# One engine makes the low halves of g: a two-layer MLP behind a dynamic convolution

## The reference

```python
w = softmax(weight_gen, axis=-1)            # (4, 4096, 8 heads, 7 taps)
x_pad = 6 zero rows + x                     # causal, x is (4, 4096, 192)
conv[s, head, :] = sum_k w[s, head, k] * x_pad[s + k, head, :]   # 24 columns per head
h = conv @ w_in                             # 192 -> 2048
g = max(0.01 * h, h)
out = g @ w_out                             # 2048 -> 192, float32
```

## Time and profile before

| | |
|---|---|
| median of 3 runs | 1031.0 us (1030.97 to 1031.47) |
| profiled execution, its own time | 1031.87 us |
| its span, first to last instruction | 1030.1 us |
| granted TensorE clock over the span | 1.000 of full speed |
| busy: TensorE, VectorE, ScalarE, GpSimd | 1020.6, 939.0, 634.3, 550.5 us |

### The profile page before, as it was taken

The page is one execution under the profiler, slowest core; times in us unless marked ns, Lnnn a source line. Parts: engine busy times, 40 slices in busy tenths (PEclk is TensorE's granted clock), DMA queues, the critical chain, the costliest instruction groups (busy, mean ns, idle before and its releaser), DMA issues.

```text
span 1030.1 us, 28954 instructions
## 1 busy us (share of the span) xinstructions
PE 1020.6 (99%) x12745; PEld 612.6 (59%) x12745; DVE 939.0 (91%) x1199; ACT 634.3 (62%) x1352; POOL 550.5 (53%) x375
## 2 busy tenths in 40 slices
PE   8999999999999999999999999999999999999998
PEld 3666655556556556655655655655565565566566
DVE  8989999999999999999999999999999999998611
ACT  7966665665556656556656555665565665566564
POOL 0114665555556655655655665565665566556543
PEclk9999999999999999999999999999999999999999
DMA  9421303112021310212112121210313112111100
GB/s 266 111 62 32 98 19 98 35 40 89 4 97 35 97 35 23 77 34 98 35 38 77 20 97 35 85 45 4 98 35 97 35 31 69 34 35 36 34 17 17
DMA packets 68309, 59.84 MB, mean 58 GB/s; under 512 B 56348, under 2 KB 60700, under 8 KB 66200
## 3 DMA queue, kind: packets, MB, share of 16 engines
q1 hardware_dynamic: 67196, 55.35, 18.4%
q0 software_dynamic: 864, 2.36, 1.3%
q10 hardware_dynamic: 124, 0.29, 0.1%
HBM read 29.34 MB, written 12.58 MB: 41 GB/s over the span
## 4 chain that ended last, share of the span: by engine, by line
PE 90%; DVE 6%; DMA 1%; ACT 1%; SPq 1%; issue 0%; POOL 0%; DVEq 0%; POOLq 0%
PE h_ps L1066 43%; PE out_ps L1176 22%; PE t_ps L1176 22%; PE out_ps L1130 1%; DVE prod L681 1%; PE h_ps L1048 1%; DMA rawO<-in_moe_w_out_dram 1%; DVE gl L883 1%; DVE conv L697 1%; PE out_ps L1140 1%; DMA prod<-prod 0%; DVE gl L755 0%; ACT g L483 0%; SPq L380 0%; ACT gh L481 0%
## 5 line engine op out<-in xcount | busy, mean ns | idle before, releaser
L349 POOL TENSOR_TENSOR gl<-g,gh 128x512 f16<-128x512 f32 x360 | 543.2, 1535 | 411.4 <-ACT g L483 411.4
L481 ACT ACTIVATE gh<-h_ps 128x512 f16<-128x512 f32 x512 | 317.6, 620 | 370.2 <-PE h_ps L1066 361.0
L1176 PE MATMUL t_ps<-wo,gh 64*128 64x384 f16 (+1 forms) x1984 | 386.6, 317 | 0.9 <-ACT gh L481 0.9
L1176 PE MATMUL out_ps<-wo,gh 64*128 64x384 f16 (+1 forms) x1984 | 386.6, 317 | 0.0
L1066 PE MATMUL h_ps<-xT,whA 64*128 64x512 f16 x1920 | 364.3, 376 | 0.0
L483 ACT ACTIVATE g<-h_ps 128x512 f32<-128x512 f32 x512 | 321.9, 629 | 0.0
L681 DVE TENSOR_TENSOR prod<-xbuf,taps 128x768 f32<-128x768 f32 x186 | 273.3, 1485 | 0.0
L697 DVE TENSOR_TENSOR conv<-conv,prod 128x768 f32<-128x768 f32 x174 | 266.4, 1531 | 1.0
L1176 PE MATMUL t_ps<-wo,gl 64*128 64x192 f16 x1920 | 233.2, 243 | 1.4 <-DVE gl L755 1.4
L1176 PE MATMUL out_ps<-wo,gl 64*128 64x192 f16 x1920 | 233.2, 243 | 0.0
L1176 PEld LDWEIGHTS t_ps<-wo,gh 64*128 64x128 f16 x1984 | 181.3, 94 | 57.6 <-ACT gh L481 1.4
(11 more groups left out here) (117 smaller groups left out, 713.3 us busy)
## 6 DMA issues: line engine op xcount, KB each, us to landing
xbuf<-in_x_dram SPq DMA_DIRECT2D x15, 1344.0 KB, 6.1
out_dram<-stage SPq DMA_DIRECT2D x31, 384.0 KB, 2.3
taps<-in_weight_gen_dram SPq DMA_DIRECT2D x16, 224.0 KB, 6.1
xT_again<-xT SPq DMA_DIRECT2D x29, 64.0 KB, 2.1
rawO<-in_moe_w_out_dram SPq DMA_DIRECT2D x4, 384.0 KB, 11.3
prod<-prod POOLq DMA_DIRECT2D x4, 384.0 KB, 4.3
rawA<-in_moe_w_in_dram SPq DMA_DIRECT2D x2, 512.0 KB, 8.6
xbuf<-in_x_dram SPq DMA_DIRECT2D x2, 384.0 KB, 7.3
```

Of the source, the lines that this page charges most:

```text
L349: nc.gpsimd.tensor_tensor(gl[:, q % RING, :], g[:, q % RING, :], gh[:, q % RING, :], ALU.subtract).then_inc(s_gl_p, 1)
L481: nc.scalar.activation(gh[:, q % RING, :], h_ps[q % GROUP][:], ACT.Prelu, alpha=SLOPE, scale=SHRINK0 if n < 2 * NG else SHRINK).then_inc(s ...
L1176: ins = nc.tensor.matmul(dst, a[rows, (m * NF + f) % RING, j * P:(j + 1) * P], moved, start=i == 0 and k < 2 and a is gh and f == 0 and pa ...
```

## The change

VectorE makes every lo in all tiles, with `group`: one subtraction of 128 x 2048 elements per group, which waits for the fourth `g` of the group. GpSimd makes none and is left with its first operations and the six adding DMAs of tiles 1 and 2. `wait_lo` now waits on one semaphore everywhere. VectorE's order from tile 2 on is rewritten: `late_tile` is gone, tile 3 and all later ones run `tile`, with tile 3 owing the rest of tile 4's convolution (operations 8 to 16) ahead of its first group; the first two softmax operations of odd tiles move from ahead of the first lo to behind `next_rows`. ScalarE's `hi_of_x(m + 1)` stands ahead of the second group in tile 2 only.

```diff
--- before.py
+++ after.py
@@ -15,7 +15,6 @@
 GROUP = 4
 RING = 3 * GROUP
 PRODS = 3
-SHARE = 4
 SLOPE = 0.01
 WARM_UP = (15, 4)
 DMA = 16
@@ -60,7 +59,8 @@
 
 CONV_TO = (4, 8, CONV.index(("top", 0)))
 CONV_EARLY = 9
-CONV_LATE = 11
+CONV_FIRST = 11
+CONV_LATE = 8
 
 
 def dynconv_mlp(nc, x, weight_gen, w_in, w_out, out):
@@ -189,7 +189,6 @@
         s_gh = sem("s_gh")
         s_g = sem("s_g")
         s_gl_v = sem("s_gl_v")
-        s_gl_p = sem("s_gl_p")
         s_out_ps = sem("s_out_ps")
         s_out_free = sem("s_out_free")
         s_out_part = sem("s_out_part")
@@ -213,13 +212,6 @@
         BY_PE = 2
 
 
-        LATE_TILES = (2, 3, 4)
-
-
-        EARLY = 2
-
-
-
         N_GROUPS = NG * TILES
         HALVES = (slice(0, P // 2), slice(P // 2, P))
 
@@ -271,11 +263,6 @@
                 engine.wait_ge(s_w_hi_v, HI_BY_VECTOR.index(piece) + 1)
             else:
                 engine.wait_ge(s_w_hi, HI_BY_SCALAR.index(piece) + 1)
-
-        def lo_on_vector(q):
-
-            return q < EARLY * NF or q % SHARE == SHARE - 1
-
 
         g_rows = g[:].rearrange("p a b -> p (a b)")
         prods0 = [g_rows[:, k * SUB * D:(k + 1) * SUB * D] for k in range(5)]
@@ -343,15 +330,6 @@
 
             for t in QUEUED_TILES:
                 add_products(t)
-
-            def lo_of_g(q, f):
-                pool.wait_ge(s_g, q + 1)
-                nc.gpsimd.tensor_tensor(gl[:, q % RING, :], g[:, q % RING, :], gh[:, q % RING, :],
-                                        ALU.subtract).then_inc(s_gl_p, 1)
-
-            for q in range(EARLY * NF, TILES * NF):
-                if not lo_on_vector(q):
-                    lo_of_g(q, q % NF)
 
         @block.sync
         def _(sp):
@@ -542,7 +520,7 @@
                     copy_out(m - 1)
                 if i == 1 and m == BY_PE:
                     exp_taps(2)
-                if i == (1 if m in LATE_TILES or m - 1 in LATE_TILES else 0) and m + 1 < TILES:
+                if i == (1 if m == BY_PE else 0) and m + 1 < TILES:
 
                     hi_of_x(m + 1)
                 if i == NG - 1 and m % 2 == 1 and m + 3 < TILES:
@@ -750,14 +728,6 @@
                 nc.vector.tensor_copy(xT_block(t % 2, 2), t2_ps[:, 0, :].rearrange("p (j c) -> p j c", c=P)
                                       ).then_inc(s_xT_v, 1)
 
-            def lo_of_g(q, f):
-                dve.wait_ge(s_g, q + 1)
-                nc.vector.tensor_tensor(gl[:, q % RING, :], g[:, q % RING, :], gh[:, q % RING, :],
-                                        ALU.subtract).then_inc(s_gl_v, 1)
-
-            def one_lo(m, f):
-                lo_of_g(m * NF + f, f)
-
             def softmax_ops(c, first, last):
                 if first == 0:
 
@@ -784,57 +754,39 @@
 
             def third_tile():
 
-                conv_ops(3, CONV_EARLY, CONV_TO[2])
-                one_lo(2, 3)
-                conv_ops(3, CONV_TO[2], N_CONV - 1)
+                m = BY_PE
+                conv_ops(m + 1, CONV_EARLY, CONV_FIRST)
+                group(m * NG)
+                conv_ops(m + 1, CONV_FIRST, N_CONV - 1)
                 softmax_ops(2, 0, 2)
-                one_lo(2, 7)
-                next_rows(2)
+                group(m * NG + 1)
+                next_rows(m)
                 softmax_ops(2, 2, N_SOFTMAX)
                 dve.wait_ge(s_softmax, N_SOFTMAX * 2)
-                conv_ops(4, 0, CONV_TO[0])
-                one_lo(2, 11)
-                conv_ops(4, *CONV_TO[:2])
-                one_lo(2, 15)
-                conv_ops(4, CONV_TO[1], CONV_LATE)
-
-            def late_tile(m):
-
-                one_lo(m, 3)
-                sums(m - 1)
-                conv_ops(m + 1, CONV_LATE if m == 3 else CONV_TO[2], N_CONV - 1)
-                if m == 4:
-                    softmax_ops(3, 2, N_SOFTMAX)
-                one_lo(m, 7)
-                next_rows(m)
-                if m == 3:
-                    softmax_ops(3, 0, 2)
-                else:
-                    dve.wait_ge(s_softmax, N_SOFTMAX * 3)
-                conv_ops(m + 2, 0, CONV_TO[0])
-                one_lo(m, 11)
-                conv_ops(m + 2, *CONV_TO[:2])
-                one_lo(m, 15)
-                conv_ops(m + 2, CONV_TO[1], CONV_TO[2] if m == 3 else N_CONV - 1)
+                conv_ops(m + 2, 0, 2)
+                group(m * NG + 2)
+                conv_ops(m + 2, 2, CONV_LATE)
+                group(m * NG + 3)
 
             def tile(m):
 
-
                 c = m // 2 + (2 if m % 2 == 1 else 1)
+                if m == BY_PE + 1:
+                    conv_ops(m + 1, CONV_LATE, N_CONV - 1)
                 if c < CHUNKS and m % 2 == 0:
                     softmax_ops(c, 2, N_SOFTMAX)
-                elif c < CHUNKS:
-                    softmax_ops(c, 0, 2)
-                one_lo(m, 3)
+                group(m * NG)
                 sums(m - 1)
                 if m + 1 < TILES:
                     next_rows(m)
-                if c < CHUNKS and m % 2 == 0:
+                if c < CHUNKS and m % 2 == 1:
+                    softmax_ops(c, 0, 2)
+                elif c < CHUNKS:
                     dve.wait_ge(s_softmax, N_SOFTMAX * c)
-                for k, f in enumerate((7, 11, 15)):
+                for k in range(1, NG):
                     if m + 2 < TILES:
-                        conv_ops(m + 2, (0, *CONV_TO)[k], CONV_TO[k])
-                    one_lo(m, f)
+                        conv_ops(m + 2, (0, *CONV_TO)[k - 1], CONV_TO[k - 1])
+                    group(m * NG + k)
                 if m + 2 < TILES:
                     conv_ops(m + 2, CONV_TO[2], N_CONV - 1)
 
@@ -975,10 +927,7 @@
             second_tile()
             third_tile()
             for m in range(3, TILES):
-                if m in LATE_TILES:
-                    late_tile(m)
-                else:
-                    tile(m)
+                tile(m)
             m, u = TILES - 1, (TILES - 1) % 2
             dve.wait_ge(s_stored[u], DMA * (m // 2))
             for j in range(2, SUB):
@@ -1109,12 +1058,7 @@
                     ins.then_inc(s_h, 1)
 
             def wait_lo(m, f):
-                if m < EARLY:
-                    pe.wait_ge(s_gl_v, m * NF + f + 1)
-                elif lo_on_vector(m * NF + f):
-                    pe.wait_ge(s_gl_v, EARLY * NF + ((m - EARLY) * NF + f) // SHARE + 1)
-                else:
-                    pe.wait_ge(s_gl_p, ((m - EARLY) * NF + f) // SHARE * (SHARE - 1) + f % SHARE + 1)
+                pe.wait_ge(s_gl_v, m * NF + f + 1)
 
             def project_hi(n):
 
```

## The result

| | before | after |
|---|---|---|
| median of 15 runs each, same chip | 1031.19 us (1030.97 to 1032.39) | 1028.69 us (1028.54 to 1031.09) |
| profiled execution: own time, span | 1031.87, 1030.1 us | 1028.63, 1026.8 us |
| ratio | | 0.9977, 95% interval 0.9969 to 0.9984 |

Forecast: 1028.5, range 1027.9 to 1031.2. The change makes the kernel 2.5 us faster. The interval does not reach 1, so the gain is clear of noise; in us it goes from 1.6 to 3.2, and the prediction's 0.2% line lies inside it.

A forecast was written before the change was run, and what follows sets the result against it. TensorE, busy 99% of the span, was taken as the bound, losing 2.75 us in step to a late VectorE. Removing stalls of 1.21 and 1.54 and adding 0.23 in tile 3 gave 1031.0 - 2.5 = 1028.5 us, range 1027.9 to 1031.2.

The forecast's parts named there:

- the prediction's 0.2% line: Smallest change that a measurement of this kernel was said to tell: about 0.2%, 2.06 us.
- The two stalls, 2.75, go: TensorE's beat loses 1.21 and 1.54 us where VectorE, slowed by GpSimd, is late; both were to vanish.
- VectorE takes all lo and still has room: With GpSimd silent, VectorE's work per tile was to take 26.9 of the 31.2 us of four beats.
- The full slot of odd tiles: VectorE's work between first and second group, tiles 5 to 27: 10.34 us, second lo late by 2.54, costing TensorE 0.
- the margin: Room before a late lo delays TensorE in odd tiles' fullest slot: predicted 0.23 us.
- G: Time when ScalarE has written a group's last `g`, from which the group's lo can start.
- the limit: Latest end of a group's lo that costs TensorE nothing: predicted 5.05 us after G.
- Rival A: The full slot is over its limit in every odd tile: 1029 to 1033 us; chance 0.23.
- Tile 3 loses 0.23: In the new order tile 3's second lo ends at G + 5.28, over 5.05; TensorE loses 0.23 us once.
- The 0.12 of a dependent operation: Extra VectorE time where an operation needs its predecessor: 0.12 us each, 0.24 of tile 3's 0.48 lateness.
- ScalarE's move costs nothing: ScalarE's hi of x one slot forward in tiles 3 to 5: 0, as it idles 0.92 us there in later tiles.
- The sum: Span 1030.1 - 1.21 - 1.54 + 0.23 = 1027.6 us; own time 1031.87 - 2.52; median 1031.0 - 2.5 = 1028.5.

The follow-up runs named there:

- old_order_groups: The changed kernel, but with VectorE's and ScalarE's orders of before; VectorE makes every lo by groups: 1034.0 us, ratio 1.0015 to before.
- share_from_6: The changed kernel until tile 5, then GpSimd shares the lo again as before from tile 6 on: 1029.85 us, ratio 0.9973 to before.
- share_till_5: The kernel before until tile 5, with VectorE making every lo from tile 6 on: 1030.12 us, ratio 0.9979 to before.
- old_order_groups_hi5: old_order_groups with ScalarE's high half of x ahead of the first group in tile 5 alone: 1030.22 us, ratio 0.9985 to before.
- gpsimd_reads: The changed kernel, with GpSimd also making its 360 subtractions on spare data nobody waits for: 1208.76 us, ratio 1.1709 to before.
- pad_80: The changed kernel with one more VectorE addition (128 x 80, step 0.15 us) in odd tiles' fullest slot: 1030.99 us, ratio 0.9988 to before.
- hi_earlier: The kernel before with only ScalarE's high half of x moved ahead of the first group in tiles 3 to 5: 1037.79 us, ratio 1.0051.

## Why the prediction was right

- **The two stalls, 2.75, go.** Right, and the cause was read right: the first, which the view of waits named as ScalarE's, was VectorE's too. old_order_groups shows it best: there the same product starts at 189.61, 0.10 after the second `stage` addition (189.10 + 0.41), and ScalarE's nearest `gh` end at 189.19 and 190.16. Before has the same 0.10 (189.44, 189.54). share_from_6 shows that changing tiles 2 to 5 is enough for the whole gain, and share_till_5 that the second stall also goes if only the tiles from 6 on are changed. old_order_groups_hi5 shows that silencing GpSimd is enough but for one line of ScalarE's order, and gpsimd_reads that the inflation of VectorE comes from GpSimd's reads.
- **VectorE takes all lo and still has room.** Right: groups start 2.20 apart from what follows, multiplies take 0.951, busy share 83% (I had said near 86).
- **The full slot of odd tiles.** Right in what it costs, nothing, but the margin was mis-sized: the lo ends at G + 4.92 against 4.82 predicted, and the limit is G + 5.02 or 5.03 against 5.05, so 0.10 is left of the 0.23. The steps between the two lo came out at 10.34 (808.05 to 818.39), and 0.02 of the predicted 10.34 was the start behind G; that start is 0.10, as in every lo of four chunks that waits. A single lo in before has 0.02. Rival A was closer than the prediction says; pad_80 shows that 0.15 more work is already too much.
- **Tile 3 loses 0.23.** Right mechanism, size 0.355. The fourth group of tile 2 has its G at 112.95 (the end of ScalarE's last `g`), and its lo started at 113.05: 0.10 behind, as wherever a lo of four chunks waits, where 0.02 was taken. From there to the next two lo are 8.28 (to 121.33) and 10.33 (to 131.66). Together 0.10 + 8.28 + 10.33 - 2 x 7.805 + 2.29 = 5.39. Of the 0.125 that the loss is over its forecast, 0.08 is that start, some 0.02 the limit, and the rest hundredths in the steps. The 0.12 of a dependent operation, without which tile 3 would lose 0.24 less, stood up: with it the slot was worked out at 8.26 without its start.
- **ScalarE's move costs nothing.** Right in after, for a reason that I didn't give: only where `x_scale` is there in time. In tile 3 of after it is done at 121.42 and ScalarE comes to it at 122.49. I had looked only at ScalarE's idle time, so here the zero was luck. Alone it costs 5 us of beats (hi_earlier), and without it the group form in the old order costs 4.2 (old_order_groups). So this edit does not stand by itself: it hangs on VectorE's order and on GpSimd's silence.
- **The sum.** Medians differ by 2.50, predicted 2.52. That they meet to 0.02 is luck: the interval of the medians is 1.6 us wide. The profiled spans differ by 3.3, as before's execution started later: its lo of group 7 starts at 84.14, after's at 83.29. From that lo to the end of the span are 945.96 and 943.51, a difference of 2.45; beats alone give 2.75 less 0.355, 2.40. That is 0.12 short of the forecast, which is tile 3's 0.125.

## What to carry to other kernels

Where two engines exclude each other, the helper's price is paid by the other engine's operations: here GpSimd took 120 x (2.20 - 0.60) = 192 us of lo from VectorE and still left it busy 83 us longer, so compare the same operation quiet and shared before giving work away. Read a loss from the beat of a periodic engine, not from the wait. When an engine becomes faster, look at the producers that it now reaches earlier. And before relying on a margin of 0.2 us, read how late an operation of the new form starts behind what it waits for; here a start taken from the old form was 0.08 short and used up a third of the margin.

## What the runs showed that I had not expected

- A GpSimd memset, which reads nothing, held VectorE operations of 128 x 4 for up to 1.2 us (0.17 quiet), and left 128 x 768 and 128 x 2048 ones with two inputs alone (950 and 2272 ns).
- 360 GpSimd subtractions that nobody waits for cost some 180 us beside a VectorE that has every lo to make (1208.76 is 176 above before on the same chip, and after is 2.5 under it), while GpSimd's 312 in share_from_6, where VectorE has only its own quarter of the lo, cost no beat.
- Giving VectorE all lo in the old order (old_order_groups) cost 4.2 us in one tile, through a wait for ScalarE.
- A VectorE multiply beside GpSimd's subtractions takes either 0.95 or 1.91 us, and a lo of four chunks starts 0.10 after its last `g` where a single one starts 0.02 to 0.04 after.
